# Four re-orderings in the opening of a fused attention and MLP kernel: a transpose bank, a pooled sum, weight roundings, a token low part

## The reference

```
out = repeat(softmax(qd kd^T) vd, 4) + softmax(masked q k^T) v      # qd, kd, vd: means of 4 rows
h   = max(x @ w1, x @ w2, x @ w3);  y = h @ w_out                   # 512 -> 768 -> 512
g   = max(0.01 * (y @ w_in), y @ w_in);  result = g @ w2_out        # 512 -> 2048 -> 512
```

## Time and profile before

| | us |
|---|---|
| median of 3 runs | 771.75 |
| lowest and highest | 770.85, 772.47 |
| the profiled execution | 771.62 |
| its span in the trace | 769.8 |
| TensorE busy in the span | 760.1 (99%) |
| VectorE, ScalarE, GpSimd busy | 448.8, 296.7, 169.5 |

### The profile page before, as it was taken

The page is one execution under the profiler, slowest core; times in us unless marked ns, Lnnn a source line. Parts: engine busy times, 40 slices in busy tenths (PEclk is TensorE's granted clock), DMA queues, the critical chain, the costliest instruction groups (busy, mean ns, idle before and its releaser), DMA issues.

```text
span 769.8 us, 13514 instructions
## 1 busy us (share of the span) xinstructions
PE 760.1 (99%) x5396; PEld 682.4 (89%) x5396; DVE 448.8 (58%) x768; ACT 296.7 (39%) x699; POOL 169.5 (22%) x212
## 2 busy tenths in 40 slices
PE   8999999999999999999999999999999999999998
PEld 7889989888888889999998888989898998889896
DVE  6877797676745453765756656564434466334433
ACT  5675545333242333433554444442222244222222
POOL 6794111211111333340435533110000000000000
PEclk9999999999999999999999999999999999999999
DMA  8733442322121023212567644446432236223402
GB/s 294 260 105 102 132 125 77 103 95 68 49 75 38 1 69 120 70 41 87 168 254 286 248 163 151 191 156 211 162 115 97 96 132 237 96 97 107 156 24 83
DMA packets 37630, 98.91 MB, mean 128 GB/s; under 512 B 2880, under 2 KB 23360, under 8 KB 34496
## 3 DMA queue, kind: packets, MB, share of 16 engines
q1 hardware_dynamic: 37568, 98.05, 36.5%
HBM read 73.92 MB, written 24.12 MB: 127 GB/s over the span
## 4 chain that ended last, share of the span: by engine, by line
PE 94%; DVE 2%; issue 1%; ACT 1%; DMA 0%; POOL 0%; SPq 0%; DVEq 0%; ACTq 0%
PE mlp_ps L1103 10%; PE mlp_ps L1105 10%; PE mlp_ps L1104 10%; PE mlp_ps L1256 8%; PE mlp_ps L1258 8%; PE mlp_ps L1257 8%; PE att_ps L1277 6%; PE att_ps L1279 6%; PE att_ps L1278 6%; PE mlp_ps L1279 3%; PE mlp_ps L1278 3%; PE mlp_ps L1277 3%; PE att_ps L1176 2%; PE att_ps L1178 2%; PE att_ps L1177 2%; PE att_ps L993 2%
## 5 line engine op out<-in xcount | busy, mean ns | idle before, releaser
L1103 PE MATMUL mlp_ps<-x_hi,wa_lo 128*128 128x288 f32 (+1 forms) x288 | 101.6, 353 | 0.3 <-DVE x_lo L1742 0.3
L1105 PE MATMUL mlp_ps<-x_hi,wa_hi 128*128 128x288 f32 (+1 forms) x288 | 97.5, 339 | 0.0
L1104 PE MATMUL mlp_ps<-x_lo,wa_hi 128*128 128x288 f32 (+1 forms) x288 | 97.2, 337 | 0.0
L1560 ACT ACTIVATE h_last_a<-wa_raw 128x384 fp32r<-128x384 f32 x72 | 37.7, 524 | 105.0 <-DVE wa_raw L1903 104.3
L1901 DVE TENSOR_TENSOR wa_raw<-mlp_ps,h_raw 128x384 f32<-128x384 f32 x24 | 13.4, 556 | 80.5 <-PE mlp_ps L1258 51.4
L1103 PEld LDWEIGHTS mlp_ps<-x_hi,wa_lo 128*128 128x128 f32 x288 | 54.1, 188 | 5.9 <-DVE x_lo L1742 0.4
L1105 PEld LDWEIGHTS mlp_ps<-x_hi,wa_hi 128*128 128x128 f32 x288 | 54.1, 188 | 4.5
L1104 PEld LDWEIGHTS mlp_ps<-x_lo,wa_hi 128*128 128x128 f32 x288 | 54.3, 189 | 4.0
L1915 DVE TENSOR_TENSOR h_last_b<-wa_raw,h_last_a 128x384 fp32r<-128x384 f32 x72 | 44.3, 620 | 23.1 <-ACT h_last_a L1560 20.9
L871 POOL TENSOR_TENSOR v_rows<-v_rows 72x512 f32<-72x512 f32 x16 | 20.4, 1275 | 152.6 <-DMA v_rows<-in_v_sum 152.6
L1279 PE MATMUL att_ps<-wa_hi,h_last_a 128*128 128x512 f32 x132 | 52.3, 396 | 0.0
(11 more groups left out here) (220 smaller groups left out, 2049.0 us busy)
## 6 DMA issues: line engine op xcount, KB each, us to landing
u_even<-u_scratch SPq DMA_DIRECT2D x8, 1792.0 KB, 7.3
u_odd<-u_scratch SPq DMA_DIRECT2D x8, 1792.0 KB, 7.1
kq_in<-in_kq SPq DMA_DIRECT2D x14, 576.0 KB, 3.8
u_scratch<-u_even SPq DMA_DIRECT2D x4, 1792.0 KB, 8.6
u_scratch<-u_odd SPq DMA_DIRECT2D x4, 1792.0 KB, 9.4
v_rows<-in_v_sum SPq DMA_DIRECT2D x16, 288.0 KB
wa_raw<-in_w SPq DMA_DIRECT2D x6, 768.0 KB, 5.9
v_win<-in_v_band SPq DMA_DIRECT2D x12, 384.0 KB, 3.6
```

The costliest lines, as they stand in the source:

```text
L1103: nc.tensor.matmul(ps, wlo, xhi, start=(n == 0), stop=False)
L1104: nc.tensor.matmul(ps, whi, xlo, start=False, stop=False)
L1105: last = nc.tensor.matmul(ps, whi, xhi, start=False, stop=(n == len(pairs) - 1))
L1560: nc.scalar.activation(g_tile(0, quad, part), g_raw[part], ACT.Copy).then_inc(g_hi_ready, 1)
```

## The change

1. `bank_of` sends `lt0` of unit 1 (its local transposes) to bank 7 (`mlp_ps3`) instead of bank 5 (`mlp_ps1`). The job before it on its bank was `av0` of unit 0 (read by VectorE line 1737); now there is none. The first value product of unit 1 on bank 5 follows `av0` of unit 0, and group 1 on bank 7 follows the transposes.
2. `XL 0 1` (the low part of token quarter 1) is ahead of `V 2` on VectorE.
3. The high parts of weight pieces 2 to 5 stand earlier, each by about one or two places, and with them GpSimd's low parts.
4. `D 6` (the sums of unit 6) stands before group 4 instead of behind group 5.

```diff
-        ("T", 2), ("N", 3), ("XH", 0, 1), ("NG", 3), ("Z", 3), ("V", 2), ("XL", 0, 1), ("W", 1, 0), ("T", 3), ("XH", 0, 2), ("XL", 0, 2),
-        ("Mk", 0, 0, 1), ("Mk", 1, 0, 1), ("Mk", 2, 0, 1), ("V", 3), ("D", 4), ("W", 1, 1),
+        ("T", 2), ("N", 3), ("XH", 0, 1), ("NG", 3), ("Z", 3), ("XL", 0, 1), ("V", 2), ("W", 1, 0), ("T", 3), ("XH", 0, 2), ("XL", 0, 2),
+        ("Mk", 0, 0, 1), ("Mk", 1, 0, 1), ("Mk", 2, 0, 1), ("V", 3), ("D", 4), ("W", 1, 1), ("W", 2, 0),
...
-        ("Mk", 0, 2, 3), ("Mk", 1, 2, 3), ("Mk", 2, 2, 3), ("X", 0, 3), ("S", 4), ("E", 4), ("W", 2, 0), ("Mk", 3, 0, 3))
+        ("Mk", 0, 2, 3), ("Mk", 1, 2, 3), ("Mk", 2, 2, 3), ("X", 0, 3), ("W", 2, 1), ("W", 3, 0), ("S", 4), ("E", 4), ("W", 3, 1), ("Mk", 3, 0, 3))
...
-    put(1.5, ("W", 2, 1))
-    for c, at in ((3, 2.4), (4, 5.4), (5, 8.4)):
+    for c, at in ((4, 1.5), (5, 3.5)):
...
-            put(s_at - (1.95 if u == PAIRS + 3 else 1.5), ("D", u + 2))
+            put(s_at - {PAIRS: 3, PAIRS + 3: 1.95}.get(u, 1.5), ("D", u + 2))
...
+    if (kind, u) == ("lt0", 1):
+
+        return BANKS + ZERO_BANK
```

## The result

| | before | after |
|---|---|---|
| median of 20 runs, us | 772.07 | 775.68 |
| lowest and highest | 770.85, 775.50 | 771.04, 781.37 |
| the profiled execution | 771.62 | 771.33 |
| its span | 769.8 | 769.5 |

The ratio is 1.0045, 95% interval [1.0024, 1.0067]: the change made the kernel slower, by 3.6 us in the median, where 771.3 was forecast. The profiled execution of the changed kernel is 0.29 us shorter than that of before. The single runs say how the two go together: four of the 20 took 771.04 to 771.35, at a mean granted clock of 0.999 to 1.000 over the span, the other sixteen 774.8 to 781.4 at 0.991 to 0.998. The profile was taken in one of the four.

The account below looks back on a forecast made before the run. TensorE was taken as the bound (94% of the chain). Gains of 0.63 and 0.31 us reach unit 4's scores; at unit 6 ScalarE's copies leave 0.53 - 0.14 = 0.39, so 771.62 becomes 771.23, median 771.3, range 770.1 to 772.6.

Parts of the forecast that it names:

- Weight roundings earlier: ScalarE's roundings of weight pieces moved forward, 0.74 us each; its idle 1.23 and 1.89 us would cover them, cost 0.
- run beside the shift of unit 4: GpSimd's earlier differences slow VectorE's shift of unit 4, delaying following steps by 0.20 us, bounds 0 and 0.6.
- The sum: At unit 6's scores 0.53 less 0.14 gives 0.39 us gained; profiled execution 771.23, median 771.3.
- The rival of starvation: GpSimd keeps the ports from quarter 1's low part from 25.70 us on; about 1.5 us slower, 773.3, chance 0.08.
- The bank: Unit 1's local transposes in bank 7 lose their 1.27 us wait; unit 3's scores begin 0.63 us sooner.
- so 0.63 carries on: The steps behind unit 3's scores follow TensorE, so the bank's 0.63 us gain is kept.
- Unit 3's division: Line 1705 on VectorE, 1.44 us beside GpSimd's value sums; might bring a further bit, counted as nothing.
- The low part ahead: Quarter 1's low part moved ahead of unit 2's sums removes a TensorE wait; gain 0.31 us.
- Unit 6's sums earlier: Sums end near 40.37 us; TensorE then waits 1.74 us for ScalarE's copy, unit 6's pooled scores 0.53 us earlier.
- The third rounding: Three roundings instead of two on ScalarE between unit 5's exponentials and unit 4's copies, with no idle time as cover.
- 0.74 us later: Delay of unit 4's copies on ScalarE relative to unit 5's exponentials, from one more rounding between them.
- The gain is eaten: Rival: blocked VectorE instructions cost 0.6 instead of 0.2 us, or roundings press; 0.39 becomes 0, 771.7, chance 0.24.

Follow-up runs that it names:

- late rows: Value rows of unit 2 ready late; forced by loading the second weight piece ahead of units 2 and 3's rows: kernel before 776.76 us, changed kernel 781.36.
- the second set: The changed kernel timed again with no edit, beside the kernel before: median 773.74 us, ratio 1.0020 [0.9990, 1.0051].
- early rows: Value rows of unit 2 loaded ahead of the first weight piece: changed kernel 771.61 us, kernel before 771.34.
- short runs: Runs of the changed kernel, unedited, in the fast group: four of 20 at 771.04 to 771.35 us, mean granted clock 0.999 to 1.000.
- long runs: The slow group of runs: in the changed kernel sixteen of 20 at 774.8 to 781.4 us; the kernel before had them up to 777.4.

## Why the prediction was wrong

**The step that failed** is "Weight roundings earlier", in the words "I cost them at 0". I asked whether ScalarE had room for them, and ahead of unit 4 it had. I followed GpSimd's differences, which start with them, only as far as "run beside the shift of unit 4", with bounds of 0 and 0.6 us. What the roundings' late place had done was to hold GpSimd back: the 3.69 us of pause in the earlier trace rows bounded how long one of VectorE's operations with two operands in SBUF could be held. Without it, and with late rows, quarter 3's low part was held for up to 8.48 us. The edit's price with late rows is 5.3 us (781.05 against 775.71, side by side). With the loads as given the whole change has a ratio of 1.0045 [1.0024, 1.0067], in the second set 1.0020 [0.9990, 1.0051], and the change without this edit 1.0003 [0.9981, 1.0025]. These come from three sets and do not settle it: there the edit's part is likely, with late rows it is shown. No run above 777 us with the loads as given has a profile, so that quarter 3's low part is what those runs wait for is taken over from the two profiles with late rows (779.44 and 781.55).

**Behind it stands a step that I did not take.** The sum was made for one execution, and its distance to the median of three runs (0.13 us) was taken for all that could differ. The wait of GpSimd for its value rows stood in the trace (1.21 us ahead of 17.26), in front of all the differences. It was a wait whose end depends on a transfer behind 768 KB of weights, and it was worth asking what happens when it ends 3 us later.

**The rival of starvation** had the right mechanism, the wrong instruction and the wrong size. It named the low part of quarter 1 in the place where edit 2 put it, at 1.5 us and a chance of 0.08. Undoing edit 2 changed nothing that six runs against five can tell (780.63 against 781.36). It was quarter 3's low part, and edit 3.

**The bank** was right in its mechanism and, at its place, in its size: no wait on 1053, a new one on line 1680, 0.62 us gained for 0.63 at unit 3's scores. But "so 0.63 carries on" failed. Unit 3's division, for which the prediction took nothing, took 1.66 us where it had taken 1.44, and unit 3's local transposes waited 0.45 us for it (0.23 before). Only 0.25 us of the gain was left at unit 3's value products. As a time the bank alone cannot be told from nothing: 1.0005 [0.9982, 1.0028].

**The low part ahead** took 0.99 us for up to 0.9 forecast, and there is no wait at 28.6. Its gain did not come on top: unit 4's scores are 0.63 us earlier, not 0.94, and with the bank alone they were 0.59 earlier (18.27 us behind unit 2's), without a wait for a low part.

**Unit 6's sums earlier** was right in that the wait went over to ScalarE's copy and became longer, 1.58 us for 1.74 forecast and 1.33 before. The third rounding was the reason, as the sum had it; two roundings fewer there brought unit 6's scores 1.15 us forward. The prediction had written this down as "0.74 us later" without asking what it was worth to undo it. It did not name the wait of 0.39 us ahead of unit 4's pooled transposes (1044), which ended with ScalarE's pooled exponentials of unit 5 by the profile. That and the 0.25 us of longer wait for the copy use up the 0.63 us.

**The sum** for the profiled execution was 0.39 us, and the profiles differ by 0.29. That they are near each other is luck: 0.21 of the 0.29 was there at unit 2's scores, and from there to unit 6's scores the change gains nothing (30.23 against 30.19 us, and with early rows 30.18 against 30.21). What came true for the short runs is the rival "The gain is eaten". The terms that were too good are the carry of the bank's gain and that of the low part. The bank alone would have kept 0.58 us there.

**Open.** What decides in a run whether VectorE gets its turn inside an unbroken row. Over 8 us were seen in two profiles (779.44 and 781.55). In four others with late rows and an unbroken row (773.55, 775.55, 775.87 and 776.39), as in the short runs, quarter 3's low part took 0.45 to 0.84 us. So the unbroken row is needed but not enough, and the exact phase was not varied. How late the rows land also differs from set to set with the same order of loads (19.1 to 22.7 us with the late order), for which no cause was looked for; nor was it measured whether the change alters how often they are late.

## What to carry to other kernels

Before moving work earlier on an engine that shares something with another, look for the pauses that its late place gave, and who used them: a pause of an engine off the critical path can be what bounds how long the critical one's operations are held. Compare two profiles from a point ahead of the first edit, not from the start of the span: here 0.21 of a difference of 0.29 us came from before it. Where a wait in the profile ends with a transfer, reprice the change with that transfer a few us later, since one profiled execution shows one draw; two loads put in another order make the bad draw happen every time, and show in one run what a median hides. The late rows themselves were the cheapest thing to mend: one load ahead of another took the kernel before from 772.82 to 771.34 in the median, and its long runs away.

## What the runs showed that I had not expected

- A VectorE subtraction of 128x288 with both inputs in SBUF took 0.45 to 0.46 us free, 3.84 us beside eight of GpSimd's differences in a row, and 8.35 and 8.48 us beside twenty. The long two ended 0.3 us behind the row, the 3.84 one shortly before the end of the eighth difference. The Trainium skill ("SBUF — State Buffer", section "Who interferes with whom") has whoever starts first hold the ports for its whole instruction while the other fully blocks. By that a wait would end after one difference, 0.58 us. These rows show fourteen: between two of GpSimd's differences the blocked instruction did not get in. In other profiles it did (0.45 to 0.84 us inside rows of 36 and 40), and with a semaphore wait between the differences it got in in both profiles (at most 0.84 and 0.85 us). So the runs do not bear out a turn after each instruction, and what decides was not found.
- The granted clock fell to 0.50 within a standstill of TensorE of 5.6 us and just behind one of 3.5 us, and the products behind them ran at 0.50 for 5.1 and 3.4 us. In other profiles with late rows the stretch at 0.50 was longer, up to 10 us (26.6 to 36.7 with the weight edit undone). Behind the wait of 1.27 us for unit 0's sums it fell in two profiles of six.
- The same transfer, issued at the same place, is ready 3 us later in some executions (17.1 against 20.1 us), and with it issued earlier the long group of runs is gone.
